# Attention with split probabilities, nine query blocks per two heads, and the sums divided out where the MLP's input is put together

## What is computed

```
scores = (q @ k.T) / sqrt(64)
scores = where(scores >= rowmax(scores) - tau, scores, -1e9)
attn   = exp(scores - rowmax(scores));  attn = attn / (rowsum(attn) + 1e-9)
x      = attn @ v, heads side by side          # [2304, 512]
h = x @ w1_in;  x = (h * clip(h + 3, 0, 6) / 6) @ w1_out      # 512 -> 2048 -> 512
h = x @ w2_in;  out = (h * sigmoid(1.702 * h)) @ w2_out
```

## Time and profile before

| | |
|---|---|
| median of 3 runs | 1228.98 us (1228.42 to 1233.22) |
| span of the profiled execution | 1225.6 us |
| TensorE matmul busy | 1184.3 us, 97%, 6408 instructions |
| VectorE busy | 525.8 us, 43% |
| ScalarE busy | 563.2 us, 46% |
| GpSimd busy | 545.1 us, 44% |
| last step of attention to first matmul of the MLP alone | 524.82 us |
| DMA | 94.29 MB, mean 77 GB/s |

### The profile page before, as it was taken

One profiled execution on the slowest core, in us unless ns is written; L12 is line 12 of the kernel. 1 busy time (PEld: TensorE's weight loads), 2 busy tenths in 40 slices (PEclk: granted clock), 3 DMA queues, 4 the chain that ended last, 5 costly groups with the idle time before them and its releaser, 6 DMA issues.

```text
span 1225.6 us, 19677 instructions
## 1 busy us (share of the span) xinstructions
PE 1184.3 (97%) x6408; PEld 1020.1 (83%) x6408; DVE 525.8 (43%) x1344; ACT 563.2 (46%) x1002; POOL 545.1 (44%) x457
## 2 busy tenths in 40 slices
PE   5999999989998999989999999999999999999998
PEld 3666677757776677789999999999999999999997
DVE  5777765576656766332222222222222322222221
ACT  5888765566645765444323333233333222222221
POOL 5888655456645565345333333224444222222222
PEclk9999999999999999999999999999999999999999
DMA  4333322141222312323233322112222112222210
GB/s 121 93 103 111 85 58 60 30 118 49 58 58 68 94 35 58 88 68 120 86 113 111 111 102 81 42 57 72 86 86 86 52 52 78 78 77 77 77 52 26
DMA packets 69736, 94.29 MB, mean 77 GB/s; under 512 B 24368, under 2 KB 45872, under 8 KB 69680
## 3 DMA queue, kind: packets, MB, share of 16 engines
q1 hardware_dynamic: 69680, 93.62, 24.8%
HBM read 70.01 MB, written 23.59 MB: 76 GB/s over the span
## 4 chain that ended last, share of the span: by engine, by line
PE 86%; DVE 4%; ACT 4%; issue 4%; POOL 0%; DMA 0%; DVEq 0%; ACTq 0%; SPq 0%; POOLq 0%
PE mm L417 19%; PE score L429 16%; PE tr L417 14%; PE score L427 12%; PE mm L403 10%; PE score L381 5%; PE tr L389 5%; PE mm L427 5%; ACT expd L663 2%; DVE neg_max L537 2%; DVE prob L551 1%; ACT w_hi L684 1%; ACT gate L702 1%; DVE act_f L580 1%; ACT x_hi L698 0%
## 5 line engine op out<-in xcount | busy, mean ns | idle before, releaser
L814 POOL TENSOR_TENSOR g_lo<-act_f,g_hi 128x384 fp32r<-128x384 f32 x192 | 193.8, 1014 | 442.8 <-ACT g_hi L710 442.8
L803 POOL TENSOR_TENSOR prob<-prob,inv_total 128x576 f32<-128x576 f32 x160 | 183.3, 1148 | 179.5 <-DVE inv_total L565 179.1
L403 PE MATMUL mm<-pt,v_raw 128*64 128x320 f32 (+1 forms) x640 | 182.4, 416 | 4.3 <-ACT o_t L678 4.3
L669 ACT ACTIVATE pt<-tr 128x640 f32<-128x640 f32 x160 | 112.3, 702 | 101.1 <-PE tr L389 100.1
L417 PE MATMUL mm<-x_hi,w_hi 128*128 128x384 f32 x432 | 149.6, 346 | 5.7 <-DVE x_lo L572 3.1
L551 DVE SCALAR_TENSOR_TENSOR prob<-score,thresh,expd 128x576 f32<-128x576 f32 x160 | 130.2, 813 | 50.4 <-ACT expd L663 43.7
L663 ACT ACTIVATE expd<-score,neg_max 128x576 f32<-128x576 f32 x161 | 118.9, 739 | 57.4 <-DVE neg_max L537 56.2
L417 PE MATMUL mm<-x_hi,w_lo 128*128 128x384 f32 x432 | 144.8, 335 | 0.0
L417 PE MATMUL mm<-x_lo,w_hi 128*128 128x384 f32 x432 | 144.7, 335 | 0.0
L537 DVE TENSOR_REDUCE neg_max<-score 128x1 f32<-128x576 f32 x161 | 121.5, 755 | 38.8 <-PE score L381 38.5
L403 PEld LDWEIGHTS mm<-pt,v_raw 128*64 128x64 f32 x640 | 77.1, 136 | 68.1 <-issue 22.0
(11 more groups left out here) (64 smaller groups left out, 2266.8 us busy)
## 6 DMA issues: line engine op xcount, KB each, us to landing
x_raw<-x_t_scratch SPq DMA_DIRECT2D x24, 768.0 KB, 5.8
q_raw<-in_qT SPq DMA_DIRECT2D x68, 144.0 KB, 2.8
k_raw<-in_kT SPq DMA_DIRECT2D x68, 144.0 KB, 2.9
stage<-in_w_in SPq DMA_DIRECT2D x16, 512.0 KB, 6.4
stage<-in_w_out SPq DMA_DIRECT2D x16, 512.0 KB, 6.5
x_t_scratch<-o_t SPq DMA_DIRECT2D x32, 144.0 KB, 2.4
part_t_scratch<-y_out SPq DMA_DIRECT2D x6, 768.0 KB, 4.2
part<-part_t_scratch SPq DMA_DIRECT2D x6, 768.0 KB, 7.8
```

Of the source, the lines that this page charges most:

```text
L403: m = pe.matmul(pv_out[0:HD, 0:n_q], v_raw[:, par, c, :], pt[:, c, cols], start=c == 0, stop=c == QB - 1)
L669: act.activation(pt[:, :, j * P:j * P + P], turned_p.rearrange("p (c n) -> p c n", c=QB), ACT.Copy).then_inc(pt_copied, 1)
L803: pool.tensor_tensor(p, p, inv_total[:, s % RING:s % RING + 1].broadcast_to([P, S]), ALU.mult).then_inc(norm_done, 1)
L814: pool.tensor_tensor(g_lo[:, c, :], act_f[:, c % 2, :], g_hi[:, c, :], ALU.subtract).then_inc(g_lo_done, 1)
```

## The change

The attention part and the mixed part are written anew, and all loops are unrolled.

- **Nine slots per two heads.** The two 64-row tails of a pair of heads share the middle slot (`MID`), whose scores are eight matmuls. 144 slots instead of 160.
- **No normalisation of probabilities.** GpSimd's multiply is gone. Masking writes over the exponent in `prob`; the row sums are inverted once per pair (`invert`), stored to memory (`store_inverse`), and multiplied in where an x tile is put together (`load_x`, `make_x` on GpSimd: add the two halves of the product, multiply by the inverse). The made tile is stored to `x1_t` for step 1.
- **Split probabilities times V.** The transposed block is written by ScalarE as `pt_hi` and by VectorE as `pt_lo` (new), V is split too (`v_hl`, high and low side by side, 128 columns of weights), and one group of queries (256 or 320 columns) is done in one slot with ten float32r matmuls.
- **Order in a slot.** VectorE: row maximum of block g+2, mask of g+1, low part of transposed block g-2. ScalarE: high part of transposed block g-2, exponent of g+2. The threshold moves to GpSimd.
- **Mixed tiles.** Step 0 uses eight tiles of 288 tokens; six of them (two per batch) are mixed in from slot 46 on, one piece of 12 matmuls a slot, with one slot in nine free (in seven for the last batch), up to slot 154, eleven slots past the last attention slot (143). Two narrow tiles, then the 18 of 384 tokens, are left for the MLP alone.

In the following rows a line is an instruction of one engine in program order. TensorE, beside the batch without MLP work, before: scores, transposes, a part of probabilities times V.

The diff, cut to its core:

```diff
+    SLOTS = 2 * FULL + 1
+    MID = FULL
+    G = PAIRS * SLOTS
...
+    GROUP_COLS = ((0, 2 * P), (2 * P, 2 * P + TAIL), (0, TAIL + 2 * P), (TAIL + 2 * P, 2 * P))
...
+    PV = {4: 0, 7: 1, 9: 2, 11: 3}
+    O_COPY = {5: 0, 8: 1, 10: 2, 12: 3}
...
+    NARROW, TT = HALF, 384
...
+    PIECES = 2 * FC
+    PIECE = {}
+    for b in range(1, B):
+        g0, every = BATCH_SLOTS * b + SLOTS + 1, 8 if b + 1 < B else 6
+        for p in range(2 * PIECES):
+            PIECE[g0 + p + p // every] = (2 * (b - 1) + p // PIECES, p % PIECES)
+    AT = {piece: g for g, piece in PIECE.items()}
+    END = max(PIECE) + 2
+
+    MAKE_X, SPLIT_X = {}, {}
+    for ti in range(MIXED + 1):
+        at = END - 8 if ti == MIXED else AT[ti, 0] - 5 if ti % 2 == 0 else AT[ti - 1, 9]
+        for k in range(KC):
+            MAKE_X[at + k], SPLIT_X[at + k + 1] = (ti, k), (ti, k)
+    MIX_ITEMS = FC + KC
...
+            def store_inverse(i):
+                sp.wait_ge(inv_done, i + 1)
+                sp.dma_start(inv_t[i].rearrange("(s p) -> p s", p=P), inv_total[:, i % 2, :],
+                             allow_slow_non_contiguous=True).then_inc(inv_stored, 16)
...
+                wait(sp, x1_stored, 16 * ti)
+                batch, col = divmod(t0, S)
+                sp.wait_ge(inv_stored, 16 * (HB // 2) * (batch + 1))
+                for ring in range(2):
+                    sp.wait_ge(o_stored[ring], 16 * (HB * (batch + 1) - (1 if ring and col == 0 else 0)))
+                rows = o_parts[HB * batch:HB * batch + HB].rearrange("(k a) p n -> a p k n", a=2)
+                for a in range(2):
+                    side = slice(a * HD, a * HD + HD)
+                    for n, buffer in ((0, x_raw), (HD, x_low)):
+                        sp.dma_start(buffer[side, :, 0:width], rows[a, n:n + HD, :, col:col + width]
+                                     ).then_inc(x_loaded, 16)
+                    inv = inv_t[KC * batch:KC * batch + KC, a * S + col:a * S + col + width]
+                    sp.dma_start(inv_b[side, :, :],
+                                 bass.AP(tensor=inv.tensor, offset=inv.offset,
+                                         ap=[[0, HD], list(inv.ap[0]), list(inv.ap[1])])).then_inc(x_loaded, 16)
+
...
-            def turn(g, s):
-                wait(pe, norm_done, g + 1)
-                wait(pe, pt_copied, g)
-                for c in range(QB):
-                    m = pe.transpose(turned_p[:, c * P:c * P + P], prob[:, s % PROBS, c * P:c * P + P], ident[:, :])
+            def turn(x):
+                pe.wait_ge(mask_done, x + 1)
+                wait(pe, pt_lo_done, x)
+                for c in range(CHUNKS):
+                    m = pe.transpose(turned_p[:, c * P:c * P + P], prob[:, x % PROBS, c * P:c * P + P], ident[:, :])
                 m.then_inc(turned, 1)
 
-            def prob_v(head, par, group, chunks):
-
-                a, b = GROUPS[group]
-                if chunks[0] == 0:
-                    wait(pe, pt_copied, QB * head + b)
-                    wait(pe, v_loaded[par], 32 * (head // 2 + 1))
-
-                    wait(pe, pv_copied, 2 * head + group)
-                cols = slice(a * P, min(b * P, S))
-                n_q = min(b * P, S) - a * P
-                for c in chunks:
-                    m = pe.matmul(pv_out[0:HD, 0:n_q], v_raw[:, par, c, :], pt[:, c, cols],
-                                  start=c == 0, stop=c == QB - 1)
-                if c == QB - 1:
-                    m.then_inc(pv_done, 1)
-
+            def prob_v(n):
+                k, side = n % 4, (n % 4) // 2
+                width = GROUP_COLS[k][1]
+                pe.wait_ge(pt_lo_done, group_last(n) + 1)
+                pe.wait_ge(v_lo_done, 2 * (n // 4) + side + 1)
+                wait(pe, o_copied, n)
+                for low, p_part in enumerate((pt_hi, pt_lo)):
+                    for c in range(CHUNKS):
+                        m = pe.matmul(pv_out[:, 0:width], v_hl[:, side, c, :], p_part[:, GROUP_BUF[k], c, 0:width],
+                                      start=low == 0 and c == 0, stop=low == 1 and c == CHUNKS - 1)
+                m.then_inc(pv_done, 1)
...
+            def mixed_piece(ti, p):
+                _, _, width = TILES[ti]
+                if p < FC:
+                    if p == 0:
+                        pe.wait_ge(x_lo_done, KC * (ti + 1))
+                        pe.wait_ge(w_lo_done, 2 * UNITS)
+                    wait(pe, mix_drained, mix_item(ti, p))
+                    h_chunk(mix_out, p, w_hi[0], w_lo[0], width).then_inc(mix_filled, 1)
+                    return
+                m, second = divmod(p - FC, 2)
+                if not second:
+                    pe.wait_ge(mix_drained, mix_item(ti, p))
+                for c in range(second * FC // 2, (second + 1) * FC // 2):
+                    if m == 0:
+                        pe.wait_ge(g_lo_done, FC * ti + c + 1)
+                    r = y_chunk(mix_out, 0, m, c, w_hi[0], w_lo[0], width)
+                if second:
+                    r.then_inc(mix_filled, 1)
+
+            pe.wait_ge(consts_done, 8)
+            scores(0)
+            scores(1)
+            for g in range(END):
+                if g + 2 < G:
+                    scores(g + 2)
+                if 0 <= g - 2 < G:
+                    turn(g - 2)
+                n = at_slot(PV, g)
+                if n is not None:
+                    prob_v(n)
+                if g in PIECE:
+                    mixed_piece(*PIECE[g])
...
+            def low_turned(x):
+                dve.wait_ge(pt_hi_done, x + 1)
+                dve.tensor_tensor(pt_place(pt_lo, x), turned_place(x), pt_place(pt_hi, x), ALU.subtract
+                                  ).then_inc(pt_lo_done, 1)
+
...
+            row_max(0)
+            row_max(1)
+            mask(0)
+            for g in range(END):
+                done = PIECE.get(g - 1)
+                if done is not None:
+                    ti, p = done
+                    if p < FC:
+                        gated(ti, mix_out, p).then_inc(mix_drained, 1)
+                    elif (p - FC) % 2:
+                        dve.wait_ge(mix_filled, mix_item(ti, p) + 1)
+                        drain_y(ti, mix_out, (p - FC) // 2).then_inc(mix_drained, 1)
+                if g + 2 < G:
+                    row_max(g + 2)
+                if g + 1 < G:
+                    mask(g + 1)
+                if 0 <= g - 2 < G:
+                    low_turned(g - 2)
+                if kind(g) == SLOTS - 1 and g < G:
+                    invert(g // SLOTS)
+                if g in SPLIT_X:
+                    low_x(*SPLIT_X[g])
...
+            for g in range(END):
+                i, s = divmod(g, SLOTS)
+                done = PIECE.get(g - 1)
+                if done is not None and done[1] < FC:
+                    act.wait_ge(mix_filled, mix_item(*done) + 1)
+                    gates(done[0], mix_out, done[1])
+                if 0 <= g - 2 < G:
+                    high_turned(g - 2)
+                if g + 2 < G:
+                    exponent(g + 2)
+                n = at_slot(O_COPY, g)
+                if n is not None:
+                    copy_o(n)
+                if done is not None and done[1] < FC:
+                    act.wait_ge(mix_drained, mix_item(*done) + 1)
+                    high_g(*done)
+                if i < PAIRS:
+                    if s == 0:
+                        high_k(2 * i + 1)
+                    if s == 1:
+                        high_v(2 * i)
+                    if s == 3 and i + 1 < PAIRS:
+                        high_q(2 * i + 2)
+                    if s == 4 and i + 1 < PAIRS:
+                        scale_q(2 * i + 2)
+                    if s == 5 and i + 1 < PAIRS:
+                        high_k(2 * i + 2)
+                    if s == 6:
+                        high_v(2 * i + 1)
+                    if s == 8 and i + 1 < PAIRS:
+                        high_q(2 * i + 3)
+                        scale_q(2 * i + 3)
+                    if s in (1, 2) and i < UNITS:
+                        high_half_unit(0, i, s - 1)
...
-            def normalize(g, s):
-
-                wait(pool, inv_done, g + 1)
-                p = prob[:, s % PROBS, 0:S]
-                pool.tensor_tensor(p, p, inv_total[:, s % RING:s % RING + 1].broadcast_to([P, S]), ALU.mult
-                                   ).then_inc(norm_done, 1)
...
+            def threshold(g):
+                r = g % RING
+                pool.wait_ge(max_done, g + 1)
+                pool.tensor_scalar(thresh[:, r:r + 1], neg_max[:, r:r + 1], -1.0, tau_abs[:, :], ALU.mult, ALU.subtract
+                                   ).then_inc(thresh_done, 1)
+
+            def make_x(ti, k):
+                width = TILES[ti][2]
+                if k == 0:
+                    pool.wait_ge(x_loaded, loads_x(ti))
+                    wait(pool, x_lo_done, KC * ti)
+                place = x_raw[:, k, 0:width]
```

(84 more changed lines are left out.)

856 lines of the change are left out of this document (389 added, 467 removed).

## The result

The changed kernel is slower: 1309.28 us, median of 4 runs (1304.71 to 1314.41), beside 1230.74 us for the kernel before (4 runs on the same chip, 1228.42 to 1233.22). The ratio is 1.0635, interval 1.0601 to 1.0669. The profiled execution took 1314.41 us, with a span of 1312.6 us; the forecast had 1192 for the span.

A forecast was written before the change was run, and what follows sets the result against it. TensorE was taken to bound the kernel (86% of the span). Of 90 us leaving it, some 56 return as slot waits: 540 for attention + 51 + 601 = 1192, plus 3.4: 1195 us, 2.8% faster; range 1172 to 1215.

The forecast's parts named there:

- the last rival: Storing 1152 four-byte values per pair makes x loads late: up to 10 us a batch, 1225 us; chance 0.06.
- Slots without MLP work: First 46 attention slots, 2.59 us each, 3.12 in the middle one; 27.1 us a pair against 24.7 before.
- the slot-8 step: At slot 8 of a pair, GpSimd's threshold comes late behind its low part; the mask waits, 2.3 us a pair.
- the first step: TensorE's probabilities times V: 11.0 us a pair of heads becomes 5.6; with fewer transposes, 94 us leave TensorE.
- Slots 46 to 144: Mixed stage: 137 us behind y pieces, 192 behind h pieces, 29 without a piece; slot 144 starts at 513.
- a slot behind an h piece: Mixed-stage slot after an MLP piece that gate and gate product follow: 4.0 us each, 48 slots, 192 us.
- one behind a y piece: Mixed-stage slot after a y piece of the MLP: 3.43 us each, 40 slots, 137 us.
- Tail: Slots 144 to 155: 18 us of work, 3 of bubbles, 6 for the late x tile; 27 us, ending at 540.
- Two narrow tiles: Start of the MLP alone, two narrow tiles before the wide ones: 51 us.
- The clock: Rival: TensorE's clock falls in the first stage, some 35 us a pair for 27.1; 1215 to 1236 us, chance 0.17.
- TensorE stays the limit: Rival: late ScalarE and GpSimd parts fall into slots with V products, mixed slots 317 us; 1130 us, chance 0.20.
- The hand-offs: Rival: engine hand-offs 0.1 us dearer each, 0.5 a slot over 144 slots, 72 us; 1267 us, slower, chance 0.12.

The follow-up runs named there:

- the run with the turned store: Changed kernel, with the inverse row sums transposed by TensorE, copied out by ScalarE and stored as nine 512-byte runs: 1229.15 us, ratio 0.9985.
- The runs on weight units and on making x: Turned-store kernel with step 1's weight units split elsewhere: ratio 0.9892; a later one with the second narrow tile's x made after the low parts of g: 0.9805.
- the last run: The run on making x, with the high parts of the odd head's q and k one slot earlier on ScalarE: 1191.80 us, ratio 0.9686.

## Why the prediction was wrong

The step that failed is the last rival, "the inverse row sums": I named the mechanism, priced it at "up to 10 us a batch, 1225", and gave it 0.06. Its size per event was near (the turn shown lost about 10 us). Wrong was how often and whom it strikes. I let it delay only the x loads that read the inverse. But the store passes the 16 DMA engines that transfers from both queues share, as the run from ScalarE's queue showed, so it holds the weights, q, k, V and output transfers issued next, once in each of 16 pairs and not once in each of three batches. As the kernel after ran, that is 78 us, 4.9 a pair; priced so, the forecast would have been 1195 + 78 = 1273, and slower. "No row shows such a transfer" was true. What I could have read was the count: 1152 values x 16 in a kernel whose page shows 69736 packets. That is 18432 more, about a quarter again, in 16 bursts on a path where weights and q, k are waited for.

The Trainium skill, "DMA: Bandwidth & Descriptors", Rules for kernel authors, says that a non-contiguous last dimension becomes one descriptor per element and should be rearranged to be contiguous. The packet counts above agree exactly (16384 between the two forms). What it costs here is 3.8 us a store in the kernel before, 4.9 in the changed one.

Step by step, the rest reads best in the run with the turned store, which removes that one fault. Exponents of ScalarE nine blocks apart there:

```profile
65.70 0.74 ACT L679 ACTIVATE prob<-score,neg_max 128x576 f32<-128x576 f32 x1
...
92.17 0.74 ACT L679 ACTIVATE prob<-score,neg_max 128x576 f32<-128x576 f32 x1
...
118.92 0.74 ACT L679 ACTIVATE prob<-score,neg_max 128x576 f32<-128x576 f32 x1
```

- *Slots without MLP work:* 26.5 and 26.8 us a pair, forecast 27.1. In the kernel after itself a pair is 85.37 - 48.28 = 37.1, of which 10 are the hold.
- *The terms.* The operations that had no row came near the values I took. Two groups of the kernel after (busy us, mean ns, idle before), then its timeline:

```profile
L573 DVE TENSOR_TENSOR pt_lo<-tr,pt_hi 128x640 fp32r<-128x640 f32 x144 | 118.2, 821 | 41.9 <-ACT pt_hi L678 41.7
L560 DVE SCALAR_TENSOR_TENSOR prob<-score,thresh,prob 128x576 f32<-128x576 f32 x144 | 116.5, 809 | 20.8 <-POOL thresh L817 20.8
```

```profile
44.80 0.29 POOL L817 TENSOR_SCALAR thresh<-neg_max,tau_abs 128x1 f32<-128x1 f32 x1
45.20 0.82 DVE L560 SCALAR_TENSOR_TENSOR prob<-score,thresh,prob 128x576 f32<-128x576 f32 x1 [2.45 <-POOL thresh L817]
...
206.30 0.84 PE L453 MATMUL mm<-pt_hi,v_hl 128*128 128x256 f32 x5
206.98 0.76 PE L453 MATMUL mm<-pt_lo,v_hl 128*128 128x256 f32 x5
```

  The low part of the transposed block takes 0.82 us as taken, the threshold 0.29 (I took 0.2, between 0 and 1.42), five V products (206.98 - 206.30) / 5 = 0.136 apart (0.133), and the mask waits 2.45 us for the threshold once a pair in the first stage, as the slot-8 step has it (2.3); with pieces the stall is 2.0 to 2.2 us in three pairs and under 0.8 elsewhere. Whole groups take 521.95 - 520.40 = 1.55 us for 320 columns and 527.44 - 526.15 = 1.29 for 256 in the turned run, so 5.7 us a pair, where the first step has 5.6.
- *Slot 46* began near 159.7 (the exponent of block 48 at 161.43, less the 1.7 of scores and row maximum); forecast 155. The x tile's inverse, loaded late (135.46, 7.85 us), stands in the chain just ahead of it, and I take it for most of the 5.
- *Slots 46 to 144:* transposes of block 142, which open slot 144, at 519.94, so 360.2 us; forecast 358. That is 3.68 us a slot against 3.65, but partly by luck. From exponent to exponent a slot behind an h piece takes 3.75 us (forecast 4.0), one behind a y piece 3.58 (3.43), and one without a piece 3.85 (2.9): I had the first too dear and the others too cheap. The schedule also has 46, 40 and 12 of them, not 48, 40 and 10.
- *Tail:* the MLP alone began at 552.02, 32 us after slot 144; forecast 27. The sum for the x load there is wrong as I worked it: 1.8 MB at the rate of rows 8 make 13.6 us, not 11. The loads took 539.17 - 527.57 = 11.6 us, so the miss is not theirs; making x took GpSimd 1.6 us a part, 6.4 for four, where I had 5.
- *Two narrow tiles:* 625.70 - 552.02 = 73.7 us; forecast 51. This second mis-sized term, 23 us, is the larger part of the 34. I took TensorE as full there, by analogy with wide tiles, and did not price that units of step 1 are loaded and split, and x is made, between GpSimd's low parts of g. The runs on weight units and on making x took 11 and 9 us out of it, and in the last run the two tiles take 597.73 - 542.30 = 55.4.
- *The clock.* In the run with the turned store the first stage is granted 0.95 and its pairs take no more than forecast, so that rival is small. In the kernel after it is at 0.83, for the most part an effect of the hold, not from the cause I gave the rival. The lower level at 22.93 us that the rival starts from the earlier trace rows was read from scores 0.24 us apart; the window of 19 to 23 us gives a granted clock of 1.00 there, so this view doesn't show the start.
- *TensorE stays the limit* did not happen: the mixed slots took 360 us and not 317, and TensorE has 72% of the chain even in the best run. *The hand-offs* did not either: mixed slots average 3.68.

So for the turned kernel: 5 + 2 + 5 + 23 = 35 us late against 1195, which is 1230 where 1229 was measured; 78 to 80 more for the store make 1309. What stays open: how the 12 us of a hold divide between the cost of a packet, its small size and the scattered write it makes; only 36-byte and 512-byte runs were tried beside 4-byte ones, and no store of few 4-byte values. That the late load of the inverse costs the 5 us before slot 46 was read from the chain and not tried by itself. Nor is it shown what the last run gained by.

## What to carry to other kernels

Count the packets of each new transfer, not its bytes: a store whose last dimension is strided went out here as one packet per value, and it delayed the loads and stores behind it from either queue. A 128xN column of per-row results goes out cheaply when TensorE turns it first, or as runs in its own layout when the reader can take them so. When work moves off the bounding engine, price the short stages between the large ones by the slowest helper engine's queue, item by item, and not by TensorE.

## What the runs showed of the hardware that was not expected

- Behind 1152 values of 4 bytes, 4.5 KB in all, the 16 DMA engines were 97% busy at 39 GB/s over 12 us; a load issued 0.6 us later took 15.28 us. As 128 runs of 36 bytes the same 4.5 KB cost 0.3 us a store in the kernel before.
- Most of the harm spreads by time, not by queue: from ScalarE's queue the kernel still took 1282.5 us of 1309.3.
- The burst can also stop the issuer: in the changed kernel SP's instructions for two loads of q lasted 6.04 us and for two of k 5.26, where two take 1.1 us with the turned store. It doesn't always: in the kernel before with the same store, the two loads of q issued behind it at 42.26 us take 1.15 us and the two of k 1.18.
